# Attention and two Strassen layers on one core: a later value load, another order of ScalarE's copies, and four roundings moved from GpSimd to ScalarE

## What is computed

```python
def _attn_ref(q, k, v, tau):            # batch 4, heads 8, sequence 576, head width 64
    scores = q @ k.T / sqrt(64)
    thresh = max(scores) - tau
    scores = where(scores >= thresh, scores, -1e9)
    attn = exp(scores - max(scores)); attn = attn / (sum(attn) + 1e-9)
    return attn @ v

x = attention output, 2304 tokens x 512
h = x @ w_in;  g = h * tanh(softplus(h));  x = g @ w_out          # layer 1, 512 -> 2048 -> 512
h = x @ w_in2; g = h * clip(h + 3, 0, 6) / 6; out = g @ w_out2    # layer 2, the same sizes
```

## Time and profile before

| | us |
|---|---|
| median of 3 runs | 1020.61 |
| all runs | 1019.88, 1020.61, 1027.29 |
| the profiled execution, one of them | 1027.29 |
| its span on the core | 1025.4 |
| outside the span | 1.9 |
| PE busy in the span | 1003.3 (98%) |
| DVE, ACT, POOL busy | 868.2, 624.6, 504.4 |

### The profile page before, as it was taken

How to read it: one execution, slowest core, us unless ns; L and a number is a source line. 1 busy time by engine, 2 the same in 40 slices (tenths; PEclk the granted TensorE clock), 3 DMA queues, 4 the chain that set the end, 5 groups by cost and what they waited for, 6 DMA issues and landing times.

```text
span 1025.4 us, 20176 instructions
## 1 busy us (share of the span) xinstructions
PE 1003.3 (98%) x6984; PEld 933.5 (91%) x6984; DVE 868.2 (85%) x1694; ACT 624.6 (61%) x1145; POOL 504.4 (49%) x512
## 2 busy tenths in 40 slices
PE   5999999999989999999999999999999999999998
PEld 4777777777768999999999999999999999999998
DVE  7899999998956899788997899877996779957884
ACT  5777777778755566456664666455564556545543
POOL 6877677678956820377006830287004840077200
PEclk9999999999989999999999999999999999999999
DMA  6589999899845889589995989453795358753675
GB/s 182 159 246 259 253 250 271 232 269 263 237 129 179 276 303 380 166 283 326 296 361 163 291 302 369 169 175 137 251 323 164 123 182 292 243 172 108 232 244 162
DMA packets 146083, 241.45 MB, mean 235 GB/s; under 512 B 11072, under 2 KB 79168, under 8 KB 145984
## 3 DMA queue, kind: packets, MB, share of 16 engines
q1 hardware_dynamic: 145984, 240.17, 72.9%
HBM read 164.76 MB, written 50.59 MB: 210 GB/s over the span
## 4 chain that ended last, share of the span: by engine, by line
PE 61%; DVE 6%; ACT 5%; DMA 4%; issue 3%; SPq 1%; DVEq 0%; ACTq 0%
PE banks L817 7%; PE banks L819 7%; PE banks L818 7%; PE banks L854 6%; PE banks L853 6%; PE banks L852 6%; PE banks L860 5%; PE banks L862 5%; PE banks L861 5%; ACT relu L1052 3%; DMA ring<-w_out_mix 2%; PE banks L732 2%; PE banks L673 2%; PE banks L694 2%; DVE first_kept L1253 1%
## 5 line engine op out<-in xcount | busy, mean ns | idle before, releaser
L1558 POOL TENSOR_TENSOR ring<-raw,ring 128x256 fp32r<-128x256 f32 x336 | 282.6, 875 | 381.3 <-ACT ring L1017 381.3
L817 PE MATMUL banks<-x_high,ring 128*128 128x384 f32 x672 | 226.9, 338 | 0.6 <-DVE first_kept L1253 0.6
L819 PE MATMUL banks<-x_high,ring 128*128 128x384 f32 x672 | 225.0, 335 | 0.0
L818 PE MATMUL banks<-x_low,ring 128*128 128x384 f32 x672 | 224.8, 335 | 0.0
L853 PE MATMUL banks<-ring,g_high 128*128 128x256 f32 x504 | 142.6, 283 | 0.0
L854 PE MATMUL banks<-ring,g_low 128*128 128x256 f32 x504 | 142.6, 283 | 0.0
L852 PE MATMUL banks<-ring,g_high 128*128 128x256 f32 x504 | 142.6, 283 | 0.0
L817 PEld LDWEIGHTS banks<-x_high,ring 128*128 128x128 f32 x672 | 126.4, 188 | 5.7 <-issue 3.8
L1173 DVE SCALAR_TENSOR_TENSOR probs<-banks,thresh,exps 128x576 f32<-128x576 f32 x144 | 117.3, 814 | 13.1 <-ACT exps L950 6.9
L818 PEld LDWEIGHTS banks<-x_low,ring 128*128 128x128 f32 x672 | 126.4, 188 | 0.0
L819 PEld LDWEIGHTS banks<-x_high,ring 128*128 128x128 f32 x672 | 126.3, 188 | 0.0
(11 more groups left out here) (115 smaller groups left out, 2130.6 us busy)
## 6 DMA issues: line engine op xcount, KB each, us to landing
ring<-w_out_mix SPq DMA_DIRECT2D x168, 512.0 KB, 4.8
raw<-w_in_mix SPq DMA_DIRECT2D x48, 896.0 KB, 6.0
w_in_mix<-prep_in SPq DMA_DIRECT2D x18, 896.0 KB, 6.0
w_out_mix<-prep_high SPq DMA_DIRECT2D x16, 896.0 KB, 5.0
w_out_mix<-prep_low SPq DMA_DIRECT2D x16, 896.0 KB, 6.9
prep_in<-w_in SPq DMA_DIRECT2D x64, 128.0 KB, 3.5
prep_out<-w_out SPq DMA_DIRECT2D x64, 128.0 KB, 2.6
k_high<-k_two_high SPq DMA_DIRECT2D x56, 144.0 KB, 3.1
```

What stands on the lines that cost most here:

```text
L817: nc.tensor.matmul(dst, w[:, 0, cols], high, start=(t == 0 and m < 4), stop=False, skip_group_check=True)
L818: nc.tensor.matmul(dst, w[:, 0, cols], low, start=False, stop=False, skip_group_check=True)
L819: mm = nc.tensor.matmul(dst, w[:, 1, cols], high, start=False, stop=(t == KH - 1), skip_group_check=True)
L1558: nc.gpsimd.tensor_tensor(ring_slot(slot)[:, 1, :], raw[q % 2][:, m, :], f32(ring_slot(slot)[:, 0, :]), ALU.subtract).then_inc(w_low_ready, 1)
```

## The change

There are three edits. SP issues `load_values(it - 1, 1)` after `load_two(it + 1, 0)` and `store_prep_in(0, it - 1)` instead of ahead of both. ACT keeps the old order of an odd step only at i = 1 and 7; at i = 3 and 5 it takes the exponentials before `keep_main`. The last four roundings of x move from POOL to ACT, after steps 2, 4, 6 and 8 of iteration 7, with the waits for `placed[2]` and `placed[3]` at the last two, and `round_w(0, 0, 0)` comes one step later, after step 16.

```diff
                 place_head(it, 1)
-                if it > 1:
-                    load_values(it - 1, 1)
                 if it + 1 < ITS:
                     load_two(it + 1, 0)
                 store_prep_in(0, it - 1)
+                if it > 1:
+                    load_values(it - 1, 1)
                 place_head(it, 2)
...
-                    if t >= PAIR_TILES:
+                    if t >= PAIR_TILES and i in (1, 7):
                         keep_main(t - 2, (s - 2) % TILES_IT, pair2)
                         take_exp(t, s)
                     else:
...
                 after(act, slot_used, slots_before(r - 1, True))
+                if r == 0 and m in (A12_B21, S4_B22):
+
+                    for k in (2, 3):
+                        act.wait_ge(placed[k], PLACED * (ITS - 1))
...
-                    if it == ITS - 1 and s == 15:
+                    if it == ITS - 1 and s in (2, 4, 6, 8):
+                        round_x(0, X_ORDER[3 + (2, 4, 6, 8).index(s)])
+                    if it == ITS - 1 and s == 16:
                         for k in range(HEADS_IT):
...
-            for n, m in enumerate(X_ORDER):
-                if n >= 3:
-                    round_x(m)
+            for m in X_ORDER:
                 rest_x(m)
```

More of the change, by code:

```diff
@@ L1529, in mix_x @@
                 nc.gpsimd.tensor_tensor(x_mix[:, m, :, :], a, b, op).then_inc(x_mixed, 1)
[L1531 to L1542, removed]
             def rest_x(m):
```

## The result

| | before | after |
|---|---|---|
| median of 4 runs each, taken together, us | 1021.2 | 1032.5 |
| lowest and highest, us | 1019.88, 1027.29 | 1030.48, 1037.07 |
| the profiled execution, us | 1027.29 | 1033.37 |
| its span, us | 1025.4 | 1031.5 |

The change makes the kernel slower: the ratio of after to before is 1.0107, with a 95% interval of 1.0062 to 1.0153. The forecast was 1023.5 us, with a range of its own of 1018 to 1030; 1032.5 lies above that and just above the 1032 at which the whole range with its rivals ends.

What follows compares the result with a forecast made beforehand. PE was taken to pace attention, SP once its slip is over. Late values 6.8, odd steps 0, roundings 1.15 and passage -5.0 sum to +2.95 us on the median 1020.6: 1023.5 us, range 1018 to 1030, with rivals 1012.5 to 1032.

Steps and rivals of the forecast that it cites:

- The wait for the values: At PE's `mix`: values landing behind the store make PE wait 3.65, 2.8 and 2.1 us in iterations 2, 4 and 6.
- The slip of 1.15 us per iteration: SP's chain: the moved value DMAs delay the rest of each iteration by 1.15 us, between 0 and 2.33.
- The sum of edit 1, 6.8 us: PE's delay at iteration 6's `mix`: 2.1 us wait plus four slips of 1.15 gives 6.7, taken as 6.8.
- rival B: SP slips its full 2.33 us an iteration and the last stop brings half clock: +11.5, or 1032 us; chance 0.13.
- Edit 2, nothing: ACT's odd steps in attention: DVE's 0.21 us wait goes, but PE's own matmuls hide it; counted 0.
- The roundings, 1.15 us: ACT in iteration 7: four added casts ahead of tail copies cost 1.15 us, between 0 and 3.3.
- The passage, -5.0 us: Passage to the layers: rounding the weights one step later removes PE's stop and half clock, winning 5.0 us, bounds 0 to 5.9.
- the difference carried to the median: After the sum: +2.95 us, reckoned on the profiled execution, was applied to the median of 1020.6, giving 1023.5 us.
- A: Attention: values arrive in time and DVE's stalls go, pace falls to 17.76 us: -7.4, or 1013 us; chance 0.2.
- C: Passage: slipped weights come after PE, their rounding still waits, 5.0 us not won: +7.95, or 1028.6 us; chance 0.12.
- The markers: Signs: value waits of 1 to 4 us, `load_two` of iteration 6 4.6 us later, tail-copy waits at most 0.7 us, full clock at the end.

Runs made afterwards that it cites:

- values_mid: Kernel before with the value DMAs issued behind the two loads but ahead of the 896 KB store: ratio 1.0061, 1027.99 us.
- store_on_act: As `values_only`, but ACT instead of SP issues the 896 KB store, after step 2: ratio 1.0093 (1.0063 to 1.0124).
- values_warm: As `values_only`, plus 20 unread PE transposes ahead of the wait for the values in iterations 2 to 6: ratio 1.0083 (1.0059 to 1.0107).
- values_only: Kernel before with only the values moved behind the loads and the store: ratio 1.0102, median 1032.62 us.
- casts_only: Kernel before with only the four roundings moved to ACT, the weights' rounding left at step 15: ratio 1.0014 (1.0005 to 1.0023).
- the second trace: Kernel before, unchanged, profiled once more: 1020.35 us, span 1018.4.
- late_only: Kernel before with only the weights' rounding moved from after step 15 to after step 16: ratio 1.0001 (0.9992 to 1.0011).

## Why the prediction was wrong

**The wait for the values (step: 4 DMAs behind the store; right in kind).** Foretold were 3.65, 2.8 and 2.1 us for iterations 2, 4 and 6, each as if nothing had shifted; the waits were 4.41, 2.12 and 2.98, and `mix` followed the last tail. The store is less than half of the cause: `values_mid` keeps 6.2 of 10.4 us of the loss without it. `store_on_act` shows that its queue is no part of it.

**The slip of 1.15 us per iteration (right).** 4.6 us were foretold for `load_two` in iteration 6, 4.9 measured. The agreement is closer than one pair of traces can show: with the values in their place this load is issued at 224.9 to 227.4 in the five traces whose program is the same up to there. That the delay is set by SP and not by the sum of PE's stops is supported by `values_warm`.

**The sum of edit 1, 6.8 us (too small, the second term that failed).** The `mix` of iteration 6 came 8.7 us later than in the earlier trace rows, 2.0 more than the 6.7 foretold: 0.3 by the slip, and 1.8 by the landing. The last value lands 240.13 - 232.65 = 7.5 us after the first was issued, where the step took 5.2 + 0.5 = 5.7, since SP needs 4.2 us to issue the four behind the store (what holds SP there, full queues by the argument, no row shows). Behind it came a half clock that was given to rival B alone: 1.2 us by the first `up` of `values_warm`, 1.7 by the share of 0.83. Together that is 9.9 to 10.4 us; `values_only` measures 10.4. This term makes the difference between the profiled executions 6.1 us in place of 2.95.

**Edit 2, nothing (right).** 0.9991, with 1 inside the interval.

**The roundings, 1.15 us (right).** `casts_only` gives 1.4.

**The passage, -5.0 us (this is the step that failed).** Against the profiled execution it came true: the `up` rows show no stop and full clock, and the delay of PE against the profile of before falls from 12.6 us at the last pair's reciprocals (L711, 294.3 against 281.7) to 307.77 - 299.87 = 7.9 at the first `up`. The error is the sentence after the sum: "the difference carried to the median". The stop of 2.66 us and the half clock behind it were those of one execution, the slowest of the three, whose raw weights were issued 2.6 us later than in the second trace and needed 6.0 us to land. The text said that this execution was 6.7 us above the median and did not ask which rows made it so. `late_only` at 1.0001 shows what the step is worth for the median: 0. Without it the same sum reads 6.8 + 1.15 = +8, or 1028.6 us. With 9.9 to 10.4 for edit 1 and 1.4 for the roundings it is 1031.9 to 1032.4, against 1032.5 measured. That it comes so close is partly luck, since medians of the kernel before alone differ by 2 us from series to series (1020.6 to 1022.8).

**The rivals.** A did not hold: the values were late. C did not hold: ACT rounds the weights without a wait. B had the time, 1032, but not for its reason: the slip was 1.2 us an iteration, not 2.33, and the clock fell to half behind stops as short as 1.80 us (iteration 6 of `values_only`), not only above 2.66. The markers that were to show the forecast right (waits of 1 to 4 us, the slip, the quiet passage) all but held, the 4.41 us aside. All of them were marks of the kernel after; none tested the base that the sum was put on.

## What to carry to other kernels

Before a stall seen in one profile is booked as a gain, hold that execution's time against the median: if it is slower by about the size of the stall, the median may not contain it, and a second profile of the same kernel decides it. Here a small transfer issued just behind or beside one of 896 KB landed late, whichever queue the large one was on, and the tails issued 1 us or more ahead of it did not. So what is wanted soonest goes first, and here it filled a wait of the issuing engine at no cost. Where one engine's program sets the pace, count the delay at its rows and not by adding up the stops it causes elsewhere.

## What the runs showed beyond expectation

- The clock falls to half behind a stop of PE of 1.80 us (iteration 6 of `values_only`; granted clock 0.89 from 235 to 250 us), and stays whole behind the 2.46 us of iteration 2 in `values_mid`. The two `mix`:

```profile
239.55 2.54 PE L732 MATMUL banks<-probsT,values 128*64 128x256 f32 x12 [1.80 <-DMA values_tail<-v]
...
87.96 1.30 PE L732 MATMUL banks<-probsT,values 128*64 128x256 f32 x10 [2.46 <-DMA values_tail<-v]
```

  The stretch from 85 to 100 us around the second:

```profile
85.00:100.00 15.00, 12.54 (x104) 9.24 (x102) 11.09 (x30) 8.98 (x16) 13.18 (x7) 1.00 0.96 258
```

  The length of one stop alone does not decide it here; what does stays open.
- Two executions of the same kernel differ by 7.0 us of span. Weights that were there 3.8 us later (2.6 by the issue, 1.2 by the transfer), with a half clock behind the wait, make 4.8 of that in the passage.
- With the values late, DVE's additions on 128x9 are held less: their median falls from the 548 ns of the earlier trace rows to 232, with the most at 1376. The one of 1.50 us in the earlier trace rows ended with GpSimd's L1518, which ran from 130.80 for 4.01 us. That is one coincidence of two rows, and whether GpSimd holds the addition was not tested by itself. In the second trace of before the median is 684. The row after:

```profile
L1193 DVE TENSOR_SCALAR totals<-sums x16: 161/232/1376, 25.2 to 308.4; 128x9 f32<-128x9 f32 x16
```

  The waits that this saves PE are small: for DVE at L705 they are 0.3 us after, 2.0 before.
